# FFN up products by Strassen's seven products, with the down products as a later stage

## The reference

```python
def _moe2_ref(x, w_gate, w_val, w_out, rms_g) -> np.ndarray:
    rms = np.sqrt(np.mean(x * x, axis=-1, keepdims=True) + 1e-06)
    xn = x / rms * rms_g
    g = xn @ w_gate                       # 2304 x 512 by 512 x 1536
    silu = g * (1.0 / (1.0 + np.exp(-g)))
    val = xn @ w_val                      # 2304 x 512 by 512 x 1536
    return (silu * val @ w_out).astype(np.float32)   # 2304 x 1536 by 1536 x 512
```

## Time and profile before

| | |
|---|---|
| median of 3 runs | 897.87 us (895.38 to 898.5) |
| the profiled execution, span from first to last instruction | 898.3 us |
| PE busy in the span | 875.0 us, 97% |
| DVE busy | 430.7 us, 48% |
| ACT busy | 294.0 us, 33% |
| POOL busy | 123.0 us, 14% |
| FFN, from its first matmul to the start of the last | 436.54 to 891.05 us |

### The profile page before, as it was taken

The page is one execution under the profiler, slowest core; times in us unless marked ns, Lnnn a source line. Parts: engine busy times, 40 slices in busy tenths (PEclk is TensorE's granted clock), DMA queues, the critical chain, the costliest instruction groups (busy, mean ns, idle before and its releaser), DMA issues.

```text
span 898.3 us, 16710 instructions
## 1 busy us (share of the span) xinstructions
PE 875.0 (97%) x6432; PEld 794.5 (88%) x6433; DVE 430.7 (48%) x875; ACT 294.0 (33%) x479; POOL 123.0 (14%) x145
## 2 busy tenths in 40 slices
PE   8999999999999999999899999999999999999996
PEld 6776859588999999999899999999999999999996
DVE  5688888997587434443456422222222222222222
ACT  4555545652356333222444321121121112112111
POOL 1010203033234221125200010010000001001001
PEclk9999999999999999999999999999999999999998
DMA  8614614021754444328633720030020002000000
GB/s 280 201 54 176 225 53 158 2 81 40 256 149 119 80 79 65 69 30 183 153 128 119 178 88 1 1 106 1 1 70 35 0 25 80 0 0 36 1 1 36
DMA packets 37185, 75.37 MB, mean 84 GB/s; under 512 B 8176, under 2 KB 24688, under 8 KB 35472
## 3 DMA queue, kind: packets, MB, share of 16 engines
q1 hardware_dynamic: 32832, 56.07, 23.5%
q0 software_dynamic: 3488, 17.85, 5.4%
q10 hardware_dynamic: 816, 0.79, 0.3%
HBM read 51.06 MB, written 23.64 MB: 83 GB/s over the span
## 4 chain that ended last, share of the span: by engine, by line
PE 85%; DVE 8%; issue 3%; ACT 2%; DMA 1%; POOL 0%; DVEq 0%; POOLq 0%; SPq 0%; ACTq 0%
PE ps L1025 11%; PE ps L1027 10%; PE ps L1026 10%; PE ps L1040 5%; PE ps L1041 5%; PE ps L1039 5%; PE ps L927 4%; PE ps L928 4%; PE ps L929 4%; PE ps L940 3%; PE ps L942 3%; PE ps L941 3%; PE ps L768 3%; PE ps L823 2%; PE ps L728 2%
## 5 line engine op out<-in xcount | busy, mean ns | idle before, releaser
L1025 PE MATMUL ps<-xnH,blkH 128*128 128x384 f32 x576 | 194.6, 338 | 3.3 <-DVE blkL L1692 2.3
L1027 PE MATMUL ps<-xnH,blkL 128*128 128x384 f32 x576 | 194.2, 337 | 0.0
L1026 PE MATMUL ps<-xnL,blkH 128*128 128x384 f32 x576 | 194.1, 337 | 0.0
L1699 DVE TENSOR_TENSOR sg<-sg,ps 128x384 f32<-128x384 f32 x72 | 39.9, 554 | 246.6 <-ACT sg L1258 246.6
L1258 ACT ACTIVATE sg<-ps 128x384 f32<-128x384 f32 x72 | 35.4, 491 | 253.2 <-PE ps L1027 253.2
L1025 PEld LDWEIGHTS ps<-xnH,blkH 128*128 128x128 f32 x576 | 108.8, 189 | 7.5 <-issue 4.7
L1026 PEld LDWEIGHTS ps<-xnL,blkH 128*128 128x128 f32 x576 | 108.9, 189 | 2.7
L1027 PEld LDWEIGHTS ps<-xnH,blkL 128*128 128x128 f32 x576 | 108.8, 189 | 0.0
L1040 PE MATMUL ps<-blkL,hH 128*128 128x512 f32 x216 | 84.9, 393 | 0.0
L1041 PE MATMUL ps<-blkH,hL 128*128 128x512 f32 x216 | 84.8, 393 | 0.0
L1039 PE MATMUL ps<-blkH,hH 128*128 128x512 f32 x216 | 84.6, 391 | 0.0
(11 more groups left out here) (219 smaller groups left out, 1552.5 us busy)
## 6 DMA issues: line engine op xcount, KB each, us to landing
stage<-in_ffn_w SPq DMA_DIRECT2D x12, 768.0 KB, 4.3
xin<-xs_dram SPq DMA_DIRECT2D x9, 578.2 KB, 9.9
xs_dram<-zrow SPq DMA_DIRECT2D x8, 578.2 KB, 8.0
qT<-in_q SPq DMA_DIRECT2D x4, 1152.0 KB, 6.5
xnH_dram<-xoH SPq DMA_DIRECT2D x8, 576.0 KB, 3.5
xnL_dram<-xoL SPq DMA_DIRECT2D x8, 576.0 KB, 4.9
xnH<-xnH_dram SPq DMA_DIRECT2D x6, 768.0 KB, 4.9
xnL<-xnL_dram SPq DMA_DIRECT2D x6, 768.0 KB, 6.3
```

Source lines behind the costliest of these rows:

```text
L1025: e.matmul(o, hi, xnH[par][:, c, :], start=(c == 0), stop=False)
L1026: e.matmul(o, hi, xnL[par][:, c, :], start=False, stop=False)
L1027: last = e.matmul(o, lo, xnH[par][:, c, :], start=False, stop=(c == KC - 1))
```

## The change

The rows are now taken as 3 groups of 768 (`NSG`), each as two halves of 384. A unit (`UNITS`, 36 in all) is one block of 128 hidden columns with one group. Gate and value of both halves of rows over two halves of the inner dimension form a 2 by 2 product of blocks; it is made of seven products (`product`, operand numbers 0 to 6) of 2 chunks by 3 parts, which is 42 matmuls of 384 columns. Four sums of rows per group (`row_sums`) and four of weights per block (`up_sums`, `up_last_sum`) are made by POOL, and the sums of products by ACT copies and DVE additions (`first_copy`, `second_copy`, `third_copy`, `first_gate`, `second_gate`, `values`). The seventh product of a unit (`last_product`) comes after the third of the next one.

The weights are outermost: the seven split operands of a block are made anew for each block (`up_high`, `up_low`), those of a group of rows once (`row_high`, `row_low`). Blocks 0 and 1 come first with groups 0 and 1, and once more at the end (as pairs 12 and 13) with group 2. x2g is stored unsplit, and loaded unsplit. The hidden rows of a unit are stored in DRAM (`hidden_out`), and the down products are a stage of their own after unit 35 (`tile`, 18 tiles of 128 rows, 36 matmuls of 512 columns each), with hidden rows loaded (`hidden_in`) and split (`tile_rows_high`, `tile_rows_low`) per tile. The FFN has no loops any more.

The diff, cut to its core:

```diff
+UNITS = ([(q, sg) for sg in range(2) for q in range(2)] + [(q, sg) for q in range(2, NF - 2) for sg in range(NSG)]
+         + [(q, sg) for sg in range(NSG) for q in (NF - 2, NF - 1)] + [(NF, NSG - 1), (NF + 1, NSG - 1)])
...
@@ sync
-                e.dma_start(xnH_dram[:, :, bass.ds(col, G)], xoH[:, :, :].bitcast(F32)).then_inc(s["xst"], 16)
-                e.dma_start(xnL_dram[:, :, bass.ds(col, G)], xoL[:, :, :].bitcast(F32)).then_inc(s["xst"], 16)
+                e.wait_ge(s["dve_xn"], n + 2)
+                e.dma_start(xn_dram[:, :, bass.ds(col, G)], x2g[:, :, :]).then_inc(s["xst"], 16)
...
             rows_out(prior)
             e.wait_ge(s["pe_s2"], total * FC + 2)
+            up_in(1)
+            group_in(1)
+            hidden_out(0)
             rows_out(last)
+            hidden_out(1)
+            e.wait_ge(s["xst"], total * 16 + 32)
+            up_in(2)
+            e.wait_ge(s["s_lo"], 7)
+            group_in(2)
...
+            up_in(3)
+            for u in range(2, NU):
+                hidden_out(u)          # waits for dve_h >= u + 1
+                if u == last_of_group(0) + 2:
+                    for third in range(3):
+                        e.dma_start(wo_st[:, third * 4:third * 4 + 4, :], ffn_out[:, third * 4:third * 4 + 4, :])\
+                            .then_inc(s[f"wo_in{third}"], 16)
+                    for n in range(2):
+                        hidden_in(n)
...
@@ tensor
+            def product(u, o, bank, fresh):
+                q, sg = UNITS[u]
+                if u == first_of_group(sg):
+                    e.wait_ge(s["s_lo"], 7 * sg + o + 1)
+                if u == first_of_pair(q):
+                    e.wait_ge(s["t_lo"], 3 * q + (1, 1, 1, 2, 2, 2, 3)[o])
...
+            def last_product(u):
+                e.wait_ge(s["dve_v"], u + 1)
+                product(u, 6, 3, False).then_inc(s["pe_D"], 1)
...
+            def unit(u):
+                product(u, 0, 0, True).then_inc(s["pe_F"], 1)
+                product(u, 1, 1, True).then_inc(s["pe_A"], 1)
+                product(u, 2, 2, True)
+                if u > 0:
+                    last_product(u - 1)
...
+                e.wait_ge(s["act_f"], u + 1)
+                product(u, 3, 0, False).then_inc(s["pe_U"], 1)
+                if u == 1:
+                    e.wait_ge(s["dve_ms"], total + 1)
...
+                product(u, 4, 3, True)
+                e.wait_ge(s["act_u"], u + 1)
+                product(u, 5, 0, False).then_inc(s["pe_V"], 1)
+            def tile(t):
+                e.wait_ge(s["d_lo"], 2 * t + 1)
...
@@ scalar
+            def up_high(q, n):
+                if n == 0:
+                    e.wait_ge(s[f"w_in{staging_of(q)}"], loads_of(q))
...
+                else:
+                    e.wait_ge(s["t_add"], 4 * q + 2 + n)
...
+            def first_sigmoid(u):
+                e.wait_ge(s["dve_a"], u + 1)
+                if u > 1:
+                    e.wait_ge(h_sem(u - 2), stores_of(u - 2))
...
+            for u in range(1, NU):
+                first_copy(u)
...
+                for q in range(2, NQ):
+                    if u == first_of_pair(q) - 1:
+                        up_high(q, 0)
+                first_sigmoid(u)
...
+                        up_high(q, 1)
+                second_sigmoid(u - 1)
+                second_copy(u)
...
+                if u == last_of_group(1) + 1:
+                    for i in range(6):
+                        out_high(i)
+                if u == last_of_group(1) + 2:
+                    for i in range(6, NF):
+                        out_high(i)
...
+                third_copy(u)
@@ vector
+            for u in range(NU):
...
+                first_gate(u)
...
+                second_gate(u - 1)
...
+                hidden_rows(u - 1)
+                values(u)
+                if u == 1:
+                    for o in range(3):
+                        row_low(1, o)
+                if u == 2:
+                    row_low(1, 6)
+                    inverse(total - 1)
+                    normal(total - 1)
...
+                if u == last_of_group(1) + 1:
+                    for i in range(6):
+                        out_low(i)
...
+                if u == NU - 1:
+                    for half in range(2):
+                        tile_rows_low(0, half)
```

More of the change, by code:

```diff
@@ L242, in build_program @@
                 "act_x2 pl_sq pl_s0 pl_ss pe_SS dve_ms act_rt dve_R",
-            "normalised, split, stored; token numbers stored, read": "dve_xn act_xh dve_xl xst idst id_in id_c",
-            "FFN weights: loaded (one per staging buffer), split (the first block's on its own)":
-                "st_0 st_1 bk_hi bk_lo pl_b",
-            "a group's rows: loaded (one per buffer)": "x_i0 x_i1",
-            "a block: up, sigmoid, products with the gate and the value, split, down":
-                "pe_V act_s dve_p dve_h act_h dve_l pe_B pe_Y",
-            "outputs: on chip, stored": "y_ev y_out",
+            "normalised, stored; token numbers stored, read": "dve_xn xst idst id_in id_c",
+            "FFN rows loaded (one per group), their sums, operands split": "x_in0 x_in1 x_in2 s_add s_hi s_lo",
+            "FFN up weights loaded (one per staging buffer), their sums, operands split":
+                "w_in0 w_in1 w_in2 t_add t_hi t_lo",
+            "a unit's products: the first, the second, sixth added, fifth added, fourth added": "pe_F pe_A pe_U pe_V pe_D",
+            "a unit's sums on chip (three), gate of rows 1, values, gate of rows 2": "act_f act_u act_v dve_a dve_v dve_c",
+            "a unit's sigmoids (two each), gated, hidden rows": "act_s dve_p dve_h",
+            "hidden rows stored (by group and buffer)": "h_o00 h_o01 h_o10 h_o11 h_o20 h_o21",
+            "FFN out weights loaded (in thirds), split": "wo_in0 wo_in1 wo_in2 wo_hi wo_lo",
+            "a tile of hidden rows loaded (one per buffer), split in halves": "h_in0 h_in1 d_hi d_lo",
+            "a tile's outputs, on chip, stored (one per buffer)": "pe_Y y_ev y_o0 y_o1 y_o2",
             "no event, see settle()": "carry_pe carry_act carry_dve carry_pool carry_sp",
@@ L1069, in _ @@
+            for u in range(NU):
+                unit(u)
+            for t in range(NT):
+                tile(t)
         @block.scalar
@@ L1275, in group @@
[L1275 to L1286 removed]
+            def up_high(q, n):
+                st, first, last = w_st[staging_of(q)], (0, 3, 1)[n], (3, 6, 2)[n]
+                to = (0, 3, 6)[n]
+                if n == 0:
+                    e.wait_ge(s[f"w_in{staging_of(q)}"], loads_of(q))
+                    if q > 1:
+                        e.wait_ge(s["pe_V"], last_of_pair(q - 2) + 1)
+                else:
+                    e.wait_ge(s["t_add"], 4 * q + 2 + n)
+                    if n == 2 and q > 1:
+                        e.wait_ge(s["pe_D"], last_of_pair(q - 2) + 1)
+                e.activation(tH_up[q % 2][:, to:to + last - first, :, :], st[:, first:last, :, :], ACT.Copy)\
+                    .then_inc(s["t_hi"], 1)
@@ L1300, in _ @@
+            second_sigmoid(NU - 1)
+            for t in range(1, NT):
+                for half in range(2):
+                    tile_rows_high(t, half)
+                y_evac(t - 1)
+            y_evac(NT - 1)
         @block.vector
@@ L1730 @@
+            second_gate(NU - 1)
+            hidden_rows(NU - 1)
+            for t in range(1, NT):
+                for half in range(2):
+                    tile_rows_low(t, half)
 def kernel(**inputs):
```

604 lines of the change are left out of this document (382 added, 222 removed).

## The result

The changed kernel takes 927.57 us (median of 4 runs, 926.04 to 928.3) against 896.65 us before (4 runs, 895.38 to 898.5): 1.034 times before, interval 1.032 to 1.036. It is slower, as forecast, but by 3.4% and not by 1.6%: 927.6 lies 2.6 us above the range of 895 to 925.

A forecast was written before the change was run, and what follows sets the result against it. PE was taken to bound the kernel. Savings of 37.6 and 5.6 us and 1.2 at the end, against 35.6, 0.5, 16.3, 1.7, 2.7 and 1.7 added, gave +14.1: span 912.4, median 912.0 us, range 895 to 925.

The forecast's parts named there:

- experts' part: Experts' steps: leaving out the split of x2g frees ACT and DVE where PE hardly waits; costed at nothing.
- a steady unit: FFN units in steady state: 7.31 us each without waits; 216 fewer matmuls in all save 37.6 us.
- wait in unit 28: Unit 28, one unit after another pair: POOL's sums come late, +0.5 us.
- waits in units 32 to 34, and at tile 0: Passage to down products: weight landings and lumped splits hold PE, +16.3 us; tile 0 waits for its row splits, +2.7.
- slow clock there, and behind tile 0's wait: PE at its lower clock after the passage's waits, +1.7 us, and again after tile 0's wait, +1.7.
- Rival D: Start: splitting hides under PE as before, costing 6 us instead of 35.6; 882 us; chance 0.14.
- rival C: One of the two long DMA waits (12.4 and 8.4 us) is absent, as SP issues earlier; 900 to 904; chance 0.10.
- rival A: Steady units also late: slow store or no spare time, some 27 units 0.7 us longer; 930 us; chance 0.10.
- rival B: Units 0 to 6: PE stays at the lower clock through the start, +12 us; 924 us; chance 0.06.
- the 12.4 us of unit 3: Unit 3's sixth product waits for x2g's store, then pair 2's weights (3.7 us load), sums and split; longest wait, 12.4 us.
- the start's 35.6: Units 0 to 6: splits, loads and norm hold PE, +35.6 us in sum, slow clock included; bounds 18 and 45.
- 2.0 us of slow clock: Start: PE's lower clock costs 2.0 us after unit 3, with a rest; earlier most falls into the next wait.

The follow-up runs named there:

- e5: Changed kernel with the last step's token numbers and their reading issued by POOL behind group 2's sums, not by SP; 1.0282 times before.
- e2: Changed kernel with the three loads of the down weights issued earlier on SP, behind hidden rows 30; 1.0258 times before.
- e3: e2 with the twelve down-weight splits spread 4, 3, 3, 2 over units 32 to 35 and tile 0's row splits moved ahead; 1.0154 times before.
- e13: e9 with eight further moves against named waits, among them the token numbers on SP between pair 2's loads and hidden rows 0; 0.9831 times before, 880.5 us.
- e1: Changed kernel with pair 2's weights in their own staging place, issued right behind group 1's rows; 1.0305 times before.
- e6: Changed kernel with e1's early weights, e5's numbers on POOL, and hidden rows 1 issued ahead of x2g's store; 1.0266 times before.
- e7: e6 with pair 3's units for groups 0 and 1 moved ahead of group 2's first unit; 1.0326 times before.
- e4: Changed kernel with SP waiting for pair 2's weights to land before issuing group 2's rows; 1.0345 times before.
- e14: e13 with only the token numbers put back behind x2g's store and ahead of hidden rows 4 on SP; 0.9876 times before.
- e9: Changed kernel with e7's order, e3's passage spread finer, and instructions ahead of named PE waits moved, numbers on POOL's queue; 0.9982 times before.
- e11: Changed kernel with the split weights of odd and even pairs exchanging places in SBUF; one run, 928.45 us.

## Why the prediction was right in direction and wrong in size

By its own steps, with the trace of the changed kernel beside them:

| step | forecast | measured |
|---|---|---|
| experts' part | nothing | last expert matmul at 431.23, 4.0 us earlier |
| first FFN matmul | 439.4 | 435.03 |
| first matmul of unit 1 | 449.2 | 448.25 |
| first matmul of unit 2 | 463.8 | 465.21 |
| start of unit 3 | 474.6 | about 477.4 (third copy of unit 2 at 477.74) |
| norm of the last rows ends | 480.9 | 483.9 |
| x2g stored | 484.6 | before 487.86 |
| weights of pair 2 landed | 488.4 | 497.7 (ACT starts on them) |
| sixth product of unit 3 | 493.3 | 502.27 |
| first matmul of unit 7 | about 522 | about 534.3 (third copy of unit 6 at 534.68) |
| a steady unit | 7.31 | 7.386 (534.68 to 719.32, 25 units; 7.36 without the 0.59 us wait) |
| wait in unit 28 | 0.5 | 0.59 |
| waits in units 32 to 34, and at tile 0 | 16.3 and 2.7 | 14.5 (8.68, 0.70, 0.30, 4.85) and 2.44 |
| slow clock there, and behind tile 0's wait | 1.7 and 1.7 | about 5 and next to nothing |
| span | 912.4 | 925.6 |

The mechanism was right: the products save what they were to save, of the steady units only unit 28 waits, as forecast, and the loss sits where it was put, in unit 3, in units 32 to 34 and at tile 0. Rival D, a start that hides everything, and rival C, one of the long waits absent, did not happen; of rival A there are 0.05 us per unit, 1.3 in all, but through no wait; rival B is there in stretches, not throughout. Of the 13.2 us between the forecast span and the real one, 12.3 are there at the start of unit 7; the start cost about 48 us, more than its upper bound of 45. The step that failed is **the 12.4 us of unit 3** within the start's 35.6, which was to be one load from a free queue and came to 18.3, and behind it the start's **2.0 us of slow clock**:

- **The queue.** The step took the weights' landing as the issue plus a duration from rows of transfers that had a free queue. Here the token numbers were issued 2.6 us ahead, and the weights landed after them. Weights: 9.8 us and not 3.7, that is 6.1 of the 12.3. e5 takes the numbers away and finds 4.0 us and a wait of 12.33. The order shown ahead of the prediction has the numbers in it, and the prediction gives them no cost; before had the same numbers behind its stores, and PE's longest wait in its FFN, 1.98 us, was for DVE and not for a transfer.
- **The way to unit 3.** Its start and the norm came 2.8 and 3.0 us late although the FFN began 4.4 us early. From unit 0 to the start of unit 2 PE waits 1.51, 2.58, 1.80 and 4.55 us. DVE's operations with two inputs in SBUF are stretched while POOL adds. In unit 0 a low part of 768 elements takes 2.40 us beside POOL's additions at 440.64 and 443.63, and 0.95 without them (DVE):

```profile
441.87 2.40 DVE L1928 TENSOR_TENSOR sL<-s_sum,sH 128x768 fp32r<-128x768 f32 x1 [0.38 <-ACT sH L1402]
...
465.85 0.95 DVE L1928 TENSOR_TENSOR sL<-s_sum,sH 128x768 fp32r<-128x768 f32 x1
```

DVE's low parts from 434.03 to unit 1's first matmul take about 5 us more than at the pace without POOL. The cleanest pair stands later: 5.31 us for the six low parts at 749.83, with POOL's sums beside them, where the six before took 3.69. The forecast priced both engines alone. GPSIMD Engine Reference of the Trainium skill, section 1 (Specifications), states that POOL shares its SBUF interfaces with VectorE for such instructions; the trace agrees (1.44 times).
- **The clock.** From 502.3 to 534.3 PE has 132 matmuls, 23.0 us at 174 ns, and waits of 1.62 and 2.63 us; 4.7 of the 32.0 us are left, at a granted clock of 0.86. All of the start was given 2.0. After the long wait 16 matmuls follow one another at 0.32 us, at the lower clock (1.2 GHz, granted 0.50), and 10 more after the wait of 2.63:

```profile
502.76:507.88 5.12, 5.12 (x17) 5.12 (x17) 4.98 (x3) 0.98 (x2) 4.96 (x3) 0.50 0.13 53
```

Ahead of unit 3 there are 36 such matmuls, 5 us more than at full clock; the forecast let most of this fall into the next wait, and how much did is not shown. At the passage there are 14 and 17, with the first of each about 5 us where 1.7 was forecast; behind tile 0's wait, where another 1.7 was forecast, the matmuls are 0.23 us apart, the pace of before, from the third on.

The forecast's terms for the waits in units 32 to 34 and at tile 0, 19.0 us in all, came to 17.0 (e2 and e3 confirm their causes). The waits also cost more than themselves: from the changed kernel to e13 PE's idle time ahead of the FFN's matmuls falls by 39.6 us (56.3 to 16.7, tile 0's 2.44 counted), the span by 48.6; the mean granted clock rises from 0.968 to 0.986. Of the other 9.0 us about 6 are PE at its lower clock (1.2 GHz): up to tile 0 the changed kernel has 93 matmuls of its FFN at 0.32 us, e13 has 52, at 0.146 us more each. The rest was not taken apart.

What the forecast left unsaid matters more to a reader: the loss against before is all order. With the order changed and no work removed, the seven products are 1.7% faster than before, not 3.4% slower. e1, e6 and e7 show that removing the longest wait alone gives little, because each hid another: the weights hid the store of hidden rows 1 (e1), that one the store of hidden rows 2 behind group 2's load (e6), and in e7 POOL's sums came late behind the numbers that it had been given. The 6.60 us wait for hidden rows 4 in e13, with 3.26 us of it reaching PE, is the largest that is left inside the units; 3.51 us stand ahead of the first FFN matmul.

## What to carry to other kernels

A transfer's landing is its place in the queue plus its duration: read on SP what is issued in the 10 us ahead of a transfer that somebody waits for, and put pieces of a few bytes where the queue is empty. Where a buffer is double and its store sits in the same queue as large loads, the store is on the path too; count its landing, not only the load's. When the longest wait is removed, ask which others ended within a few us of it, and expect no more than the distance to the next.

## What the runs showed of the hardware

- 288 pieces of 4 bytes from DRAM to DRAM took about 10 us on SP's queue with nothing issued behind them and the last load 2.8 us ahead (e13: issued 435.05, the reading that waits for them issued 445.52), 7.8 in e14, and 7.0 to 8.2 on POOL's (e5, e7, e9). What stood behind them on SP's queue landed 5 us late or more: e4's weights took 9.0 us and not the 4.0 of e5, e1's hidden rows 11.2 and not the median of 2.7, and e14's hidden rows were waited for 5.1 us longer than e13's. On POOL's queue they still delayed SP's: in e9 issued by POOL at 534.55, hidden rows 8 were waited for 7.06 us. SP in e13:

```profile
435.05 0.62 SPq L557 DMA_DIRECT2D ids_dram<-xs_dram  x1
445.52 0.41 SPq L613 DMA_DIRECT2D idF<-ids_dram  x1
```

DMA: Bandwidth & Descriptors of the Trainium skill, section "Issuing engines are not separate DMA queues", says that all queues end on the same 16 engines; e9 agrees. In e5 the numbers were issued later as well, at 512.59, when nobody waited; no run changes the queue alone.
- Where the split weights lie in SBUF changes PE's pace by 1.8% (7.28 to 7.41 us for 42 matmuls and their weight loads), with no wait and at full clock (granted 1.00 from 534.3 to 727). e11 shows that it is the place; why, no run tells.
